# Fused attention and two feed-forward layers on one core: weight parts in the last step of a pair, attention outputs joined by GpSimd, low parts of the first tokens on VectorE

## What is computed

```python
q_bits = (np.einsum('bhsd,dk->bhsk', q, proj) > 0).astype(np.int64)
k_bits = (np.einsum('bhsd,dk->bhsk', k, proj) > 0).astype(np.int64)
...
mask = q_bucket[:, :, :, None] == k_bucket[:, :, None, :]
scores = scale * np.matmul(q, k.transpose(0, 1, 3, 2))
scores = np.where(mask, scores, -1000000000.0)
scores = scores - np.max(scores, axis=-1, keepdims=True)
attn = np.exp(scores)
attn = attn / (np.sum(attn, axis=-1, keepdims=True) + 1e-09)
return np.matmul(attn, v).astype(np.float32)
...
gate = 1.0 / (1.0 + np.exp(-(x @ w_gate)))       # first layer, 512 -> 1536 -> 512
val = x @ w_val
return (gate * val @ w_out).astype(np.float32)
...
h = x @ w_in                                     # second layer, 512 -> 2048 -> 512
g = np.where(pos, h, np.where(neg, 0.0, (h + beta) ** 2 / (4.0 * beta)))
return (g @ w_out).astype(np.float32)
```

## Time and profile before

| what | value |
|---|---|
| median of 3 runs | 824.1 us (823.56 to 824.25) |
| profiled execution | 823.15 us, of which 821.2 us span from first to last instruction |
| granted TensorE clock | 0.998 of full (2.4 GHz) |
| busy share of the span | PE 98%, VectorE 47%, ScalarE 47%, GpSimd 28% |
| pairs 1 to 6, 39.7 to 220.25 us (180.55 us) | PE 177.22, VectorE 153.95, ScalarE 150.83, GpSimd 113.43 us busy |
| last pair up to its last step, 220.25 to 247.64 us (27.39 us) | PE 24.35, VectorE 20.74, ScalarE 23.88, GpSimd 19.61 us busy |
| 271.42 us to the end (549.8 us) | PE 545.50 us busy |

### The profile page before, as it was taken

The page is one execution under the profiler, slowest core; times in us unless marked ns, Lnnn a source line. Parts: engine busy times, 40 slices in busy tenths (PEclk is TensorE's granted clock), DMA queues, the critical chain, the costliest instruction groups (busy, mean ns, idle before and its releaser), DMA issues.

```text
span 821.2 us, 10609 instructions
## 1 busy us (share of the span) xinstructions
PE 801.9 (98%) x4015; PEld 685.2 (83%) x4015; DVE 382.0 (47%) x633; ACT 389.4 (47%) x623; POOL 230.1 (28%) x236
## 2 busy tenths in 40 slices
PE   6999999999999999999999999999999999999998
PEld 5898898898988788888888888888888888888886
DVE  4888888888875321232121312125433543344333
ACT  3788888888886332121111323234433433344332
POOL 2556666566675635000000033432100000000000
PEclk9999999999999999999999999999999999999999
DMA  7894685485300532000000013320000100010001
GB/s 166 168 211 100 142 161 114 88 162 131 107 1 1 154 116 64 27 1 0 1 1 1 0 50 105 102 78 26 1 0 1 52 1 1 1 52 0 1 1 51
DMA packets 62242, 50.10 MB, mean 61 GB/s; under 512 B 28640, under 2 KB 51888, under 8 KB 62064
## 3 DMA queue, kind: packets, MB, share of 16 engines
q1 hardware_dynamic: 62032, 49.42, 24.8%
q10 hardware_dynamic: 160, 0.00, 0.0%
HBM read 27.27 MB, written 3.15 MB: 37 GB/s over the span
## 4 chain that ended last, share of the span: by engine, by line
PE 80%; POOL 7%; ACT 5%; DVE 3%; issue 3%; DMA 1%; SPq 1%; POOLq 0%; ACTq 0%
PE ps L562 17%; PE ps L564 17%; PE ps L563 17%; PE ps L686 5%; PE ps L687 5%; PE ps L688 5%; PE ps L540 4%; POOL probs L411 2%; PE ps L555 2%; PE ps L556 2%; PE ps L528 2%; PE ps L531 2%; ACT body L724 2%; DVE body L957 2%; PE ps L493 1%
## 5 line engine op out<-in xcount | busy, mean ns | idle before, releaser
L562 PE MATMUL ps<-xh,arena 128*128 128x512 f32 x480 | 186.8, 389 | 0.0
L564 PE MATMUL ps<-xh,arena 128*128 128x512 f32 x480 | 186.8, 389 | 0.0
L563 PE MATMUL ps<-xl,arena 128*128 128x512 f32 x480 | 186.8, 389 | 0.0
L418 POOL TENSOR_TENSOR arena<-stage,arena 128x1024 fp32r<-128x1024 f32 (+1 forms) x26 | 73.6, 2841 | 246.2 <-ACT arena L753 246.2
L1008 DVE TENSOR_TENSOR gate<-ps,gate 128x512 f32<-128x512 f32 x36 | 24.9, 691 | 200.6 <-ACT gate L815 200.6
L957 DVE TENSOR_TENSOR body<-ps,body 128x768 fp32r<-128x768 f32 x96 | 91.2, 952 | 31.4 <-ACT body L724 30.6
L564 PEld LDWEIGHTS ps<-xh,arena 128*128 128x128 f32 x480 | 90.1, 188 | 18.7
L562 PEld LDWEIGHTS ps<-xh,arena 128*128 128x128 f32 x480 | 90.1, 188 | 18.7
L563 PEld LDWEIGHTS ps<-xl,arena 128*128 128x128 f32 x480 | 90.1, 188 | 18.6
L815 ACT ACTIVATE gate<-ps 128x512 f32<-128x512 f32 x36 | 21.5, 598 | 176.3 <-PE ps L564 176.3
L728 ACT ACTIVATE probs<-probs,small 128x768 f32<-128x768 f32 x96 | 89.9, 937 | 19.2 <-DVE probs L946 19.0
(11 more groups left out here) (92 smaller groups left out, 1179.5 us busy)
## 6 DMA issues: line engine op xcount, KB each, us to landing
stage<-in_moe_w_out_dram SPq DMA_DIRECT2D x28, 256.0 KB, 3.4
body<-qh SPq DMA_DIRECT2D x15, 384.0 KB, 5.3
body<-kh SPq DMA_DIRECT2D x30, 192.0 KB, 5.3
stage<-in_moe_w_in_dram SPq DMA_DIRECT2D x16, 256.0 KB, 2.8
qn<-in_q_dram SPq DMA_DIRECT2D x16, 192.0 KB, 4.6
kn<-in_k_dram SPq DMA_DIRECT2D x16, 192.0 KB, 5.8
body<-ql SPq DMA_DIRECT2D x16, 192.0 KB, 5.5
vn<-in_v_dram SPq DMA_DIRECT2D x16, 192.0 KB, 2.5
```

What stands on the lines that cost most here:

```text
L562: pe.matmul(dst, wh, ah, start=start, stop=False)
L563: pe.matmul(dst, wh, al, start=False, stop=False)
L564: return pe.matmul(dst, wl, ah, start=False, stop=stop)
```

## The change

Four edits. (1) The odd halves up to j = 27 are joined as the even ones are: ScalarE copies both parts, GpSimd adds them, at u3 and u9 as well as at u0 and u6. (2) The last three halves (29, 30, 31; 29 and 31 were so before) are copied and added by ScalarE and VectorE. TensorE and the others wait for the new semaphore `o_last`, or for `o_copied`, in place of `o_added`. (3) `split_part` stands at u11 instead of u8. (4) `low_x0` moves from GpSimd (u5 to u8) to VectorE (u4 to u7).

```diff
-        o_ready, o_copied, o_done, o_added = sem("o_ready"), sem("o_copied"), sem("o_done"), sem("o_added")
+        o_ready, o_copied, o_done, o_last = sem("o_ready"), sem("o_copied"), sem("o_done"), sem("o_last")
+        LATE = 2 * NH - 3
...
@@ GpSimd
-                pool.wait_ge(o_done, j // 2 + 1)
+                pool.wait_ge(o_done, j + 1)
...
-                if g % T == 0 and 12 <= g < STEPS:
+                if g % HT == 0 and 12 <= g < STEPS:
                     add_half((g - 12) // HT, g - HT + 1)
                 if g < STEPS and g % T == 2:
                     split_v(g // T)
                 if u == late(i) + 5 and i < NP - 1:
                     scale_codes(i + 1)
-                if 1 <= i < 7 and u == 8:
+                if 1 <= i < 7 and u == 11:
                     split_part(i - 1)
-                if i == NP - 1 and 5 <= u < 5 + KT:
-                    low_x0(u - 5)
             add_half(2 * NH - 4, STEPS)
-            add_half(2 * NH - 2, STEPS)
@@ TensorE
                 if i > 1 and not keys:
-                    pe.wait_ge(o_added, 2 * (i - 1) - 1)
+                    pe.wait_ge(o_copied, 4 * (i - 1) - 2)
...
-                    if j > 1:
-                        pe.wait_ge(o_added if j % 2 else o_copied, j // 2 if j % 2 else j - 1)
+                    if j - 2 >= LATE:
+                        pe.wait_ge(o_last, j - 1 - LATE)
+                    elif j > 1:
+                        pe.wait_ge(o_copied, j - 1)
...
-            pe.wait_ge(o_copied, 2 * NH - 1)
+            pe.wait_ge(o_last, 2)
             up1(0, 0, (1,))
-            pe.wait_ge(o_added, NH)
+            pe.wait_ge(o_last, 3)
             up1(0, 1, (1,))
@@ ScalarE
             def copy_other(j):
                 lo = D * (j // 2 % 2)
-                if j % 2:
-                    return
                 if j:
-                    act.wait_ge(o_done, j // 2)
+                    act.wait_ge(o_done, j)
                 act.copy(o_part[lo:lo + D, :], o_bank(j)[lo:lo + D, :]).then_inc(o_copied, 1)
...
-            copy_half(2 * NH - 2)
-            copy_other(2 * NH - 2)
+            copy_last(2 * NH - 2)
@@ VectorE
+            def low_x0(c):
+                dve.wait_ge(xh_ready, c // 2 + 1)
+                last = dve.tensor_tensor(xl[:, c:c + 1, :], group_x(0, c, 1), xh[:, c:c + 1, :].bitcast(F32),
+                                         ALU.subtract)
...
-                if g % T == 2 and g >= 14:
-                    add_half((g - 11) // HT)
+                if i == NP - 1 and 4 <= u < 4 + KT:
+                    low_x0(u - 4)
...
-            add_half(2 * NH - 1)
+            add_last(2 * NH - 2)
+            add_last(2 * NH - 1)
```

More of the change, by code:

```diff
@@ L436, in copy_top @@
                 pool.wait_ge(first_tops, n + 1)
[L438 to L443, removed]
             def add_half(j, after):
@@ L637, in down1 @@
                 if f == 0 and g == 0:
-                    pe.wait_ge(o_done, NH)
-                    pe.wait_ge(o_added, NH)
+                    pe.wait_ge(o_done, LATE)
+                    pe.wait_ge(o_last, 3)
                 elif f == 0:
@@ L734, in copy_half, with copy_last @@
                 act.wait_ge(o_ready, j + 1)
-                first = act.copy(x_half(j), o_bank(j)[D - lo:2 * D - lo, :])
-                if j % 2:
-                    first.then_inc(o_copied, 1)
+                act.copy(x_half(j), o_bank(j)[D - lo:2 * D - lo, :])
+            def copy_last(j):
+                lo = D * (j // 2 % 2)
+                act.wait_ge(o_ready, j + 1)
+                act.copy(x_half(j), o_bank(j)[D - lo:2 * D - lo, :]).then_inc(o_copied, 1)
             def copy_other(j):
                 lo = D * (j // 2 % 2)
-                if j % 2:
-                    return
                 if j:
-                    act.wait_ge(o_done, j // 2)
+                    act.wait_ge(o_done, j)
                 act.copy(o_part[lo:lo + D, :], o_bank(j)[lo:lo + D, :]).then_inc(o_copied, 1)
@@ L782, in _ @@
                             act.wait_ge(coded[(NP - 1) % 2][xx], all_coded(NP - 1, xx))
-                        act.wait_ge(o_done, NH // 2)
-                        act.wait_ge(o_added, NH // 2)
+                        act.wait_ge(o_done, NH)
                     act.copy(xh[:, 2 * u - 2:2 * u, :], group_x(0, 2 * u - 2)).then_inc(xh_ready, 1)
@@ L787, in _ @@
             high_probs(STEPS - 4)
-            copy_half(2 * NH - 3)
-            copy_other(2 * NH - 3)
+            copy_last(2 * NH - 3)
             high_probs(STEPS - 3)
@@ L798, in _ @@
                 high_w(f)
-            copy_half(2 * NH - 1)
-            copy_other(2 * NH - 1)
+            copy_last(2 * NH - 1)
             def high_x(g, n, used, done, which=(0, 1)):
@@ L820, in group1 @@
                     if g == 0 and f == 0:
-                        act.wait_ge(o_done, NH)
-                        act.wait_ge(o_added, NH)
+                        act.wait_ge(o_done, LATE)
+                        act.wait_ge(o_last, 3)
                     if g == 0 and f + EARLY + 2 < T1:
@@ L958, in low_probs, with add_last @@
                                   ph[j % 2][:, :, cols].bitcast(F32), ALU.subtract).then_inc(pt_split, 1)
-            def add_half(j):
+            def low_x0(c):
+                dve.wait_ge(xh_ready, c // 2 + 1)
+                last = dve.tensor_tensor(xl[:, c:c + 1, :], group_x(0, c, 1), xh[:, c:c + 1, :].bitcast(F32),
+                                         ALU.subtract)
+                if c % 2:
+                    last.then_inc(xl_ready, 1)
+            def add_last(j):
                 lo = D * (j // 2 % 2)
                 dve.wait_ge(o_copied, j + 1)
-                dve.tensor_tensor(x_half(j), o_bank(j)[lo:lo + D, :], x_half(j), ALU.add).then_inc(o_added, 1)
+                dve.tensor_tensor(x_half(j), o_bank(j)[lo:lo + D, :], x_half(j), ALU.add).then_inc(o_last, 1)
             def low_x(g, n, high, done, which=(0, 1)):
@@ L996, in _ @@
             low_probs(STEPS - 4)
-            add_half(2 * NH - 3)
+            add_last(2 * NH - 3)
             low_probs(STEPS - 3)
```

## The result

The changed kernel takes 815.5 us (median of 4 runs, 814.26 to 817.56) against 824.17 us of the kernel before (4 runs, 823.56 to 824.59): ratio 0.9898, 95% interval 0.9876 to 0.9919. The profiled execution took 815.21 us with a span of 813.3 us; that of before 823.15 and 821.2.

A forecast was written before the change was run, and what follows sets the result against it. TensorE sets the pace, stalled by VectorE's add and GpSimd's weight part at u8. Five pairs 4.75, pair 6 with the last pair 1.3, join 0.5: 6.6 us off 824.1, 817.5 us; range 814.3 to 821.3.

The forecast's parts named there:

- The pairs: Pairs 1 to 6: stalls at u10 and u11 go, about 0.55 before q's transposes stays; gain 0.95 us a pair.
- The last pair up to u5: Last pair, u0 to u5: starts 0.95 us early, ScalarE's new copy at u2 eats 0.5, u5 0.46 earlier.
- The last pair from u5 to u11: Last pair: six steps of 2.07 us plus 1.6 plus 0.8; u11 starts 1.3 us earlier than before.
- the 0.8: Last pair: VectorE's four subtractions wait for GpSimd instructions in progress at three of the four, 0.8 us in all.
- The 1.6: Last pair: with a subtraction VectorE needs 2.46 us a step against TensorE's 2.07; 4 x 0.39 = 1.6 us.
- The join: Stretch after attention: one ScalarE copy less for half 30 lets GpSimd's low parts and VectorE's `hl` end earlier, 0.5 us gained.
- C: Rival: a new wait eats half, from late sums at u0 (820.2 us) or subtractions waiting whole scalings (820.3 us); chance 0.13.
- That cover: Pairs, u0: GpSimd's sums come before VectorE asks for them, with only 0.1 to 0.2 us to spare.
- E: Rival: slower, ScalarE's added copies make u9's high part late and stand before u11; +6.0, 830.1 us; chance 0.10.
- B: Rival: ScalarE is not late, so the wait before q goes too; 6 x 0.5 more, 814.5 us; chance 0.10.

The follow-up runs named there:

- run 1: The changed kernel with the weight parts (`split_part`) back at u8 instead of u11: 821.66 us, ratio 0.9976 to the kernel before; a pair 30.02 us.
- run 2: The kernel before with only the weight parts moved from u8 to u11: 820.37 us, ratio 0.9954 to the kernel before; a pair 29.51 us.
- run 3: The changed kernel with weight parts back at u8 and `low_x0` back on GpSimd, leaving only the halves' edits: 824.16 us, ratio 1.0006 to the kernel before.
- run 7: The changed kernel with the adds of the odd halves of u8 back on VectorE: 817.4 us, ratio 0.9925 to the kernel before; a pair 29.42 us.
- run 9: The changed kernel with the adds of the odd halves of u2 back on VectorE: 814.99 us, ratio 0.9898 to the kernel before; a pair 29.09 us.
- run 5: The changed kernel with the first tokens' low parts (`low_x0`) back on GpSimd at u5 to u8: 818.24 us, ratio 0.9926 to the kernel before.
- run 6: The changed kernel with half 30 as before (ScalarE copies both parts, GpSimd adds): 815.98 us, ratio 0.9905 to the kernel before; join 23.75 us.
- run 10: The changed kernel with ScalarE's copy of a half put behind the high part at u11 alone: 816.39 us, ratio 0.9910 to the kernel before.
- run 8: The changed kernel with ScalarE's copy of a half put behind the same step's high part in every third step: 821.84 us, ratio 0.9977 to the kernel before.
- run 11: The changed kernel with first tokens' high parts copied by GpSimd at u5, VectorE's four subtractions spread over u6, u8, u10, u11: 814.04 us, ratio 0.9883 to before.

## Why the prediction was right, and where it was off

The forecast was 6.6 us faster, 817.5 us; measured were 8.7 by the medians (8.4 by the ratio, 6.7 to 10.2 by its interval) and 7.9 between the traces. The mechanism came as forecast; the sum is low since several terms were taken too dear, all in the same direction. Only the 0.45 us lost at the start and behind the join go the other way.

- **The pairs.** Forecast 0.95 us a pair, measured 1.08 (6.5 in six). The chain (evacuation early, reciprocals early, low part of u9 now behind ScalarE, no wait at u10 and u11, one of some 0.5 before q) is what the rows show. Laid over the kernel before with u10 in the same place (3.14 us later), the low part of u9 starts at 155.67 (forecast 155.67), that which frees the slot for q at 159.91 (159.92), and the transposes of q at 160.98 (161.0). Runs 1 to 3 and 7 show that both causes were needed. Two things were small: u10 and u11 gave 0.97, and u3 gave 0.09 that I had put at nothing ("VectorE's add there ended as late as the copy will"; it ended 0.19 later, see run 9). That the other pairs repeat pair 4 within 0.05 us was read wrongly for pair 1, which takes 29.78 us before and 28.69 in the change; its gain, 1.09, is that of the others.
- **The last pair up to u5.** Forecast: 0.5 of the lead eaten by ScalarE's copy at u2; measured 6.29 - 6.02 = 0.27 (u5 at 225.89 instead of 231.91). Run 9, which has no second copy at u2, wins it back: u0 to u5 takes 11.65 us, 11.93 in the change and 11.66 before.
- **The last pair from u5 to u11.** Forecast 12.4 + 1.6 + 0.8 = 14.8 us, measured 239.96 - 225.89 = 14.07. The term that was too large is the 0.8 for VectorE waiting for GpSimd: beside the undisturbed 0.67 the four took 0.3 us more in all, and GpSimd's instructions took 0.9 us more, where it had room. I had a GpSimd instruction in progress at three of the four; there was one at two, with 0.34 and 0.21 us left to run. The 1.6 can't be split off in the rows. VectorE's rounds with a subtraction took 2.55, 2.50, 2.35 and 2.49 us, about the 2.46 of the forecast, but TensorE felt only part of it: beside run 5, where the subtractions are GpSimd's, its steps u6 to u9 are 1.1 us longer. So the last pair gave 1.4 us, and pair 6 ahead of it 1.1; the forecast had 1.3 for both together.
- **The join.** Forecast 0.5, measured 0.48, and 0.45 by run 6, each with GpSimd's two low parts of the weights earlier or later by as much.
- **The rivals.** C did not come: the sums at u0 kept their cover of 0.14 us, and the subtractions waited for no whole instruction. That cover was forecast at 0.1 to 0.2 and is thin, as run 10 shows. E, the slower one, did not come either: the high part of u9 ended where it was forecast (155.64 in the place of 155.63). But its engine was rightly named. ScalarE's copy and high part stand ahead of VectorE's low parts at u9 and u11, and in between ScalarE waits 0.20 us for VectorE's evacuation once. B was not to be had by the edits tried (runs 8 and 10).

The stretch behind the join is 0.25 us longer than before. This is not tied to the edits: over the fourteen traces it takes 549.8 us in eight, among them runs 5, 6, 7 and 9, which are built from the change, and 550.1 in six. What makes the two lengths is open. The difference between the medians' 8.7 and the traces' 7.9 is within the scatter.

## What to carry to other kernels

When an engine stalls behind two late helpers in turn, undoing one may show nothing: read what the waiting engine would meet next before judging an edit worthless, and try both. Put filler work where the helper's next customer is furthest away, counted in the order in which the customer asks. And when the wait that is left stands behind an engine that has run nearly without a gap for several steps, expect that reordering within that engine moves the wait. The two reorderings here (runs 8 and 10) did so and cost time; taking work off the engine helped in the last pair (run 11), and was not tried in pairs 1 to 6.

A figure that comes out within its range is not yet a mechanism: run 3's last pair did so, and the step lengths show another cause than the one expected.

## What the runs showed of the hardware

VectorE and GpSimd delay each other when VectorE's instruction has both inputs in SBUF: 0.69 us alone, 1.33 and 1.34 against two long GpSimd instructions in progress. VectorE's end is then a fixed time behind that of the GpSimd instruction: 0.55 us in the kernel before, in the change and in run 6 at the join, and 0.55 and 0.54 at two subtractions of the last pair. So what VectorE loses is the rest of the GpSimd instruction less some 0.13 us (0.69 or 0.67 less the 0.55). VectorE's instructions with one input in PSUM lost nothing against the same two at the join (0.56 and 0.69 us, as elsewhere).

What I had not expected is how uneven the price is in the last pair: there the four subtractions came through with 0.3 us of delay in all, and three GpSimd rows that overlap them were 0.17, 0.32 and 0.43 us longer than their kind. Where VectorE had started first (230.05 and 232.55), GpSimd was the one that took longer. And where GpSimd had two scalings one behind the other (the row of 234.20), VectorE got in between them: it waited for the first, and the second waited for it. The Trainium skill ("SBUF — State Buffer", section SBUF: two separate sides) says that of a VectorE instruction with two SBUF inputs and a GpSimd instruction that reads SBUF, the one that starts first keeps the access for its whole instruction and the other waits. The rows of this case agree. So the engine that an edit has just loaded need not be the one that pays.
